# Three edits to the first batch of a fused attention, token-mixer and channel-mixer kernel

## The reference, cut to what matters

```python
for t in range(S):                                  # attention, per batch and head
    state = alpha[:, :, t, :, None] * state + np.einsum('bhd,bhe->bhde', k[:, :, t], v[:, :, t])
    y[:, :, t] = np.einsum('bhd,bhde->bhe', q[:, :, t], state)

xt = x.transpose(0, 2, 1)                           # token mixer, then channel MLP
h = np.maximum(xt @ w_tok1, 0.0) @ w_tok2
u = x + h.transpose(0, 2, 1)
x = u + np.maximum(u @ w_ch1, 0.0) @ w_ch2

xk = mu_k * x + (1.0 - mu_k) * x_prev               # channel mix, x_prev is x one token earlier
xr = mu_r * x + (1.0 - mu_r) * x_prev
k = np.maximum(xk @ w_k, 0.0)
out = 1.0 / (1.0 + np.exp(-(xr @ w_r))) * (k * k @ w_v)
```

## Time and profile before

| | before |
|---|---|
| median of 3 runs | 732.86 us (732.38 to 733.08) |
| the profiled execution | 732.64 us |
| its span in the trace | 730.9 us |
| PE busy | 725.4 us (99%) |
| DVE busy | 472.2 us (65%) |
| ACT busy | 331.1 us (45%) |
| POOL busy | 197.2 us (27%) |

### The profile page before, as it was taken

How to read it: one execution, slowest core, us unless ns; L and a number is a source line. 1 busy time by engine, 2 the same in 40 slices (tenths; PEclk the granted TensorE clock), 3 DMA queues, 4 the chain that set the end, 5 groups by cost and what they waited for, 6 DMA issues and landing times.

```text
span 730.9 us, 13853 instructions
## 1 busy us (share of the span) xinstructions
PE 725.4 (99%) x4556; PEld 719.3 (98%) x4556; DVE 472.2 (65%) x1298; ACT 331.1 (45%) x953; POOL 197.2 (27%) x344
## 2 busy tenths in 40 slices
PE   9999999999999999999999999999999999999998
PEld 8999999999999999999999999999999999999998
DVE  7988888865888875888883412446457365473561
ACT  5866544432544442444442332436346264373550
POOL 3875564333243331334432440310000000000000
PEclk9999999999999999999999999999999999999999
DMA  9973535542425544243531224010011010110000
GB/s 205 220 153 77 97 56 108 85 72 65 56 42 86 103 82 77 49 55 56 111 62 33 87 86 141 33 33 34 33 54 44 33 38 28 52 43 32 11 22 32
DMA packets 210187, 50.90 MB, mean 70 GB/s; under 512 B 190416, under 2 KB 207312, under 8 KB 210128
## 3 DMA queue, kind: packets, MB, share of 16 engines
q1 hardware_dynamic: 206992, 45.05, 30.9%
q0 software_dynamic: 1152, 4.72, 1.8%
q10 hardware_dynamic: 1984, 0.41, 0.3%
HBM read 37.17 MB, written 12.98 MB: 69 GB/s over the span
## 4 chain that ended last, share of the span: by engine, by line
PE 96%; SPq 1%; DMA 1%; DVE 1%; ACT 0%; issue 0%; DVEq 0%
PE bank L798 21%; PE bank L814 21%; PE bank L894 14%; PE bank L872 14%; PE bank L881 5%; PE bank L716 5%; PE bank L684 4%; PE bank L786 3%; PE bank L755 3%; PE bank L721 2%; PE bank L714 2%; PE bank L679 1%; SPq L351 1%; PE bank L767 1%; PE bank L692 1%; PE bank L656 1%
## 5 line engine op out<-in xcount | busy, mean ns | idle before, releaser
L991 ACT ACTIVATE hid_hi<-bank 128x384 fp32r<-128x384 f32 x96 | 47.2, 492 | 115.5 <-PE bank L798 115.2
L1257 DVE SCALAR_TENSOR_TENSOR hid_lo<-bank,hid_hi 128x384 fp32r<-128x384 f32 x96 | 53.2, 555 | 65.5 <-ACT hid_hi L991 64.5
L1091 ACT ACTIVATE relu_k<-bank 128x384 f32<-128x384 f32 x64 | 31.5, 492 | 106.0 <-PE bank L872 86.1
L798 PE MATMUL bank<-u_hi,wch_hi 128*128 128x384 f32 x288 | 72.1, 358 | 0.0
L798 PE MATMUL bank<-u_lo,wch_hi 128*128 128x384 f32 x288 | 66.3, 338 | 0.0
L814 PE MATMUL bank<-hid_lo,wch_hi 128*128 128x384 f32 x288 | 65.5, 334 | 0.0
L798 PE MATMUL bank<-u_hi,wch_lo 128*128 128x384 f32 x288 | 65.4, 334 | 0.0
L814 PE MATMUL bank<-hid_hi,wch_hi 128*128 128x384 f32 x288 | 65.4, 334 | 0.0
L814 PE MATMUL bank<-hid_hi,wch_lo 128*128 128x384 f32 x288 | 65.4, 334 | 0.0
L1391 DVE TENSOR_TENSOR x_half<-bank,x_half 128x384 f32<-128x384 f32 (+2 forms) x25 | 13.5, 541 | 77.4 <-PE bank L894 75.3
L567 POOL TENSOR_SCALAR_AFFINE_SELECT relu_k<-relu_k 128x256 f32<-128x256 f32 x72 | 29.3, 407 | 112.2 <-ACT relu_k L973 112.2
(11 more groups left out here) (141 smaller groups left out, 1833.3 us busy)
## 6 DMA issues: line engine op xcount, KB each, us to landing
w_raw<-in_moe_w_ch SPq DMA_DIRECT2D x12, 384.0 KB, 3.6
x_scratch<-x_half POOLq DMA_DIRECT2D x8, 576.0 KB, 3.6
out<-x_half SPq DMA_DIRECT2D x23, 192.0 KB, 1.9
vt<-in_v SPq DMA_DIRECT2D x48, 72.0 KB, 2.3
x_scratch<-x_sum SPq DMA_DIRECT2D x18, 192.0 KB, 2.1
x_sum<-x_scratch SPq DMA_DIRECT2D x72, 48.0 KB, 2.2
qka<-in_q SPq DMA_DIRECT2D x49, 48.0 KB, 2.2
qka<-in_alpha SPq DMA_DIRECT2D x49, 48.0 KB, 2.2
```

The costliest lines, as they stand in the source:

```text
L798: mm = nc.tensor.matmul(dst, ch1_w(a, n % KC, jj), u[c][:, n % KC, half * HT:(half + 1) * HT], start=(n == 0), stop=(n == 3 * KC - 1))
L991: nc.scalar.activation(dst, b_ring[t % 2][:, 0:HT], func).then_inc(tile_hi, 1)
L1257: ins = nc.vector.scalar_tensor_tensor(dst, src, 0.0, hi, ALU.max, ALU.subtract)
```

## The change

1. **Start.** Alpha of the first pair is the first load on SP, k the second; q of the first pair is the first on ACT's queue. PE turns alpha first, into a bank of its own, and signals it (`first_alpha_done`); the two scans of step 0 wait for this alone. Two fill passes stand between alpha's transpose and those of q and k. The fill is made of transposes in place of products, with new counts.
2. **Weights.** The 20 half pieces are spread over the slots 4 to 25 (none in 11 and 19), and POOL's whole pieces stand in slots 5, 7, 9, 12, 14, 16, 18, 21, 23 and 25. SP loads piece 1 ahead of chunk 2. The loads of mu and DVE's use of them move behind the head and the batches.
3. **x^T of the first token half of batch 0** goes through DRAM: SP stores three groups of rows in slot 16 and loads the blocks of one group in each of slots 20, 21 and 22 (four transfers each); DVE turns them in slots 25 to 27 and adds them in `down_base`. The nine PE transposes of this half are gone. The second half stays as it was. The loads of batch 1's first half block are spread over slots 16 to 19, and those of the second stand behind the loop and mu.

```diff
+        def transposed_alpha(r, i):
+            return bank[2][0:W2, 0:P] if is_first(r) and i == 0 else transposed_qka(r, i)[:, 2 * P:3 * P]
...
+        def half_slot(j):
+            return FIRST_UNIT + (STEPS - 1) * j // (2 * CH1_END)
         def pieces_in(s):
-            bounds = [min(max(n - 3, 0) * CH1_END // (STEPS - NP), CH1_END) for n in (s, s + 1)]
-            return range(*bounds)
+            return [n for n in range(CH1_END) if half_slot(2 * n + 1) == s]
...
+            def store_first_x():
+                sp.wait_ge(xlo_ready, NP * TM)
+                for m in range(KC):
+                    sp.dma_start(x_rows[0][m].rearrange("(c p) f -> p c f", p=P),
+                                 x_sum[:, 0:TM, m * P:(m + 1) * P]).then_inc(first_rows_stored, 16)
+            def load_first_x_blocks(m):
+                sp.wait_ge(first_rows_stored, 16 * KC)
+                for a in range(4):
+                    sp.dma_start(x_sum[32 * a:32 * (a + 1), m, :].rearrange("p (n j) -> p n j", j=32),
+                                 x_rows[0][m].rearrange("(n p) (a j) -> a p n j", p=32, j=32)[a])\
+                      .then_inc(first_raw_loaded[m], 16)
...
-            for n, t in ((0, q), (2, alpha)):
+            for n, t, loaded in ((2, alpha, alpha_pair_loaded), (1, k, pair_loaded)):
...
-            for c in range(1, 3):
-                load_qka(c)
-                load_piece(c - 1)
-                load_v(c)
+            load_qka(1)
+            load_piece(0)
+            load_v(1)
+            load_piece(1)
+            load_qka(2)
+            load_v(2)
             load_piece(2)
-            for n, m in enumerate((mu_k, mu_r)):
...
-                if s % NP == 0 and s >= NP * (NC - 2) and s < STEPS:
-                    load_half(1, s // NP - NC + 2)
-                if s % NP == 3 and s >= NP * (NC - 2) and s < STEPS:
-                    load_half_v(1, s // NP - NC + 2)
+                n = s - NP * (NC - 2)
+                if n == 0:
+                    store_first_x()
+                if 0 <= n < 3:
+                    load_half(1, 0, (n,))
+                elif n == 3:
+                    load_half_v(1, 0)
+                elif 4 <= n < 4 + KC:
+                    load_first_x_blocks(n - 4)
                 for n in pieces_in(s):
                     load_piece(n + NRAW)
+            for n, m in enumerate((mu_k, mu_r)):
+                sp.dma_start(mu[:, n, :], m.rearrange("(c p) -> p c", p=P),
+                             allow_slow_non_contiguous=True).then_inc(mu_loaded, 16)
+            load_half(1, 1)
+            load_half_v(1, 1)
...
-            WARM = (4, 4, 2, 3, 2, 1, 1)
+            WARM = (8, 5, 2, 6, 4, 2, 2)
...
-                for n in range(3):
+                for n in (2, 0, 1):
+                    if i == 0 and n == 0:
+                        pe.wait_ge(pair_loaded, 32)
...
+                    if i == 0 and n == 2:
+                        mm.then_inc(first_alpha_done, 1)
+                        keep_warm(2)
...
-                if b == 0:
+                turned_by_pe = b == 0 and half == 1
+                if turned_by_pe:
...
-                    nc.tensor.matmul(b_ring[1][:, 0:P], ident[:, :], ident[:, :], start=True, stop=True)
+                    nc.tensor.transpose(b_ring[1][:, 0:P], ident[:, :], ident[:, :])
...
-                n, half = divmod(s - 3, 2)
-                if 0 <= n < CH1_END:
-                    split_half_hi(n, half)
+                for j in range(2 * CH1_END):
+                    if half_slot(j) == s:
+                        split_half_hi(*divmod(j, 2))
...
+            def turn_first_x(m):
+                dve.wait_ge(first_raw_loaded[m], 64)
+                nc.vector.transpose(x2_half[0][:, m, :], x_sum[:, m, :]).then_inc(first_turned, 1)
...
-                if b == 0:
+                if b == 0 and half == 0:
+                    dve.wait_ge(first_turned, m + 1)
+                    ins = nc.vector.tensor_tensor(x2_half[0][:, m, :], src, x2_half[0][:, m, :], ALU.add)
+                elif b == 0:
                     ins = nc.vector.tensor_copy(x2_half[half][:, m, :], src)
...
+                if STEPS + 1 <= s <= STEPS + KC:
+                    turn_first_x(s - STEPS - 1)
```

More of the change, by code:

```diff
@@ L177, in attention_mixer_channel_mix @@
         omu_ready = sem("omu_ready")
+        alpha_pair_loaded = sem("alpha_pair_loaded")
         pair_loaded = sem("pair_loaded")
@@ L184, in attention_mixer_channel_mix @@
         w_lo_ready = sem("w_lo_ready")
+        first_alpha_done = sem("first_alpha_done")
         tr_done = sem("tr_done")
@@ L214, in attention_mixer_channel_mix @@
         x_turned = sem("x_turned")
+        first_rows_stored = sem("first_rows_stored")
+        first_raw_loaded = [sem(f"first_raw_loaded{n}") for n in range(KC)]
+        first_turned = sem("first_turned")
         x2_stored = [sem(f"x2_stored{n}") for n in range(2)]
@@ L359, in load_v, with load_half @@
                              v[0, :, c * P:(c + 1) * P, :].rearrange("h p d -> p h d")).then_inc(v_loaded[buf], 16)
-            def load_half(r, n):
+            def load_half(r, n, tensors=range(3)):
                 buf = buffers(r, TM * n)[0]
@@ L370, in load_half @@
                     sp.wait_ge(turned, TM * (before - 1))
-                for a, t in enumerate((q, k, alpha)):
+                for a in tensors:
                     for lane, h, d0, d1, f0 in GROUPS:
                         sp.dma_start(blocks[buf][lane:lane + 32, a, :, f0:f0 + d1 - d0],
-                                     t[r, 2 * p + h, ts, d0:d1].rearrange("(t p) d -> p t d", p=32))\
+                                     (q, k, alpha)[a][r, 2 * p + h, ts, d0:d1].rearrange("(t p) d -> p t d", p=32))\
                           .then_inc(qka_loaded[buf], 16)
@@ L410, in load_piece @@
                 sp.dma_start(dst.rearrange("p (k n) -> p k n", k=piece_size(n)[0]), PIECES[n][0]).then_inc(loaded, 16)
-            for n, t in ((0, q), (2, alpha)):
+            for n, t, loaded in ((2, alpha, alpha_pair_loaded), (1, k, pair_loaded)):
                 sp.dma_start(qka3[0][n][:, 0:2, 0:D], t[0, 0:2, 0:P, :].rearrange("h p d -> p h d"))\
-                  .then_inc(pair_loaded, 16)
+                  .then_inc(loaded, 16)
             sp.dma_start(qka3[0][0][:, 2:H, 0:D], q[0, 2:H, 0:P, :].rearrange("h p d -> p h d"))\
@@ L649, in transposes @@
                     pe.wait_ge(consts_v, 2)
-                    pe.wait_ge(pair_loaded, 48)
+                    pe.wait_ge(alpha_pair_loaded, 16)
                 if i % NP == (1 if i < NP else 0):
@@ L654, in transposes @@
                     pe.wait_ge(qkd_ready, i - 1)
-                for n in range(3):
-                    mm = nc.tensor.transpose(
-                        transposed_qka(r, i)[:, n * P:(n + 1) * P], qka3[qb][n][:, 2 * p:2 * p + 2, :].rearrange("p h d -> p (h d)"), ident[:, :])
+                for n in (2, 0, 1):
+                    if i == 0 and n == 0:
+                        pe.wait_ge(pair_loaded, 32)
+                    dst = transposed_alpha(r, i) if n == 2 else transposed_qka(r, i)[:, n * P:(n + 1) * P]
+                    mm = nc.tensor.transpose(dst, qka3[qb][n][:, 2 * p:2 * p + 2, :].rearrange("p h d -> p (h d)"),
+                                             ident[:, :])
+                    if i == 0 and n == 2:
+                        mm.then_inc(first_alpha_done, 1)
+                        keep_warm(2)
                 mm.then_inc(tr_done, 1)
@@ L786, in token_down @@
                     mm = nc.tensor.matmul(dst, h1[i][:, kt, m * P:(m + 1) * P], tok2_w(j, kt, half),
-                                          start=(b > 0 and n == 0), stop=(n == 3 * KT - 1))
+                                          start=(n == 0 and not turned_by_pe), stop=(n == 3 * KT - 1))
                 mm.then_inc(tile_done, 1)
@@ L1047, in mix_next @@
                         mix_step(nxt, half, n, 0, KC - 1)
-            act.dma_start(qka3[0][1][:, 0:2, 0:D], k[0, 0:2, 0:P, :].rearrange("h p d -> p h d"))\
+            act.dma_start(qka3[0][0][:, 0:2, 0:D], q[0, 0:2, 0:P, :].rearrange("h p d -> p h d"))\
                .then_inc(pair_loaded, 16)
-            for n, t in ((1, k), (2, alpha)):
+            for n, t in ((2, alpha), (1, k)):
                 act.dma_start(qka3[0][n][:, 2:H, 0:D], t[0, 2:H, 0:P, :].rearrange("h p d -> p h d"))\
@@ L1140, in scans @@
             def scans(r, i):
-                alphaT = transposed_qka(r, i)[:, 2 * P:3 * P]
+                alphaT = transposed_alpha(r, i)
                 if i >= 4:
                     dve.wait_ge(state_sum, NST * r + updates(r, i - 3))
-                if is_first(r):
+                if is_first(r) and i == 0:
+                    dve.wait_ge(first_alpha_done, 1)
+                elif is_first(r):
                     dve.wait_ge(tr_done, i + 1)
@@ L1156, in scale_qk @@
                 G = STEPS * r + i
+                if is_first(r) and i == 0:
```

(7 more changed lines are left out.)

2 lines of the change are left out of this document (removed).

## The result

The changed kernel takes 736.53 us (735.70 to 737.83, 6 executions) against 732.97 us for the kernel before (732.38 to 733.91): ratio 1.0049, 95% interval 1.0039 to 1.0059. It is slower by 0.5%, 3.6 us. The forecast was 732.4 with a range up to 734.8, so the time lies outside it. The profiled execution took 737.53 us, with a span of 735.8; it is one of the three with the lowest mean granted clock (0.995, 736.78 to 737.83 us), and the other three, at 0.997 and 0.998, took 735.70 to 736.28. So the trace shows more of the loss (4.9 us against the profiled execution of before) than the median has.

What follows compares the result with a forecast made beforehand. DVE was taken to bound the head until about 51 us, PE from there on. The terms -0.14 - 0.32 + 0.95 - 0.99 = -0.50 us took 732.86 to 732.4 us, range 731.0 to 734.8.

Steps and rivals of the forecast that it cites:

- the paragraph on x^T: End of the head: three transpose triples leave PE, -0.99 us; DVE's turns fit its 2.08 us wait, loads in time, cost 0.
- x^T lands late: Rival, end of the head: third group lands at 56, PE waits about 1 us more, +0.5, 733.4 us; chance 0.09.
- the clock rises late: Rival, slots 2 to about 6: transposes delay the fast clock, 733.6 to 735.6 us; chance 0.21, or 0.03 slow throughout head.
- The start: Step 0's scans start earlier, step 1 still waits for all of chunk 0; shorter PE fill before the first mask: -0.14 us.
- The weights: Spread of weight halves in the head: -0.32 us for DVE's stall, +0.95 for POOL's late low part.
- The stall near 17 us: DVE's state update at 17.39 starts at 17.07, as ACT's half of piece 1 moves a slot later: -0.32 us.
- POOL's last low part: End of the head: step 23's low part, behind later weight pieces, ends at 54.8 in place of 53.84: +0.95 us.
- The transposes: Three triples of x^T transposes leave PE's stream in `token_down`: -0.99 us, bounded from below by 0.6.
- the sum of -0.50: Whole kernel: start -0.14, stall -0.32, POOL +0.95 and transposes -0.99 us added together, chance 0.53.

Runs made afterwards that it cites:

- e3_fill_gap: The changed kernel with 24 more fill transposes on PE between the first token product and the next scores: 734.70 us, ratio 1.0026 to the kernel before.
- e5_late_products: e2_turn_late with the fill made of products in place of transposes, about as many passes: 732.66 us, ratio 0.9998 to the kernel before.
- e7_start_only: The kernel before with the first edit (start) alone: 732.84 us, ratio 0.9996 to the kernel before.
- e10_xt_only: The kernel before with the third edit (x^T through DRAM) alone: 736.30 us, ratio 1.0033 to the kernel before.
- e2_turn_late: The changed kernel with DVE's third turn moved behind the low parts of q and h and slot 1's work: 732.48 us, ratio 0.9995 to the kernel before.
- e1_no_xt: The changed kernel with its third edit undone, x^T of the first half from PE's transposes again: 733.37 us, ratio 1.0008 to the kernel before.
- e4_old_spread: The changed kernel with the weight halves back in slots 3 to 22: 734.45 us, ratio 1.0029 to the kernel before.
- e9_quiet_landing: The changed kernel with the two 384 KB weight loads behind the third group's blocks waiting for the turns: 736.34 us, ratio 1.0036 to the kernel before.

## Why the prediction was wrong

**The step that failed** is the paragraph on x^T: "They must not wait for their data", with its estimate that the third group's loads "are issued around 49 to 51 us and land 2.2 later", at 53, and "nothing is lost". They were issued from 52.38 to 54.38 and landed at 57.5. Of the 4.5 us, some 3.4 are SP's line: I counted it from 35 us with every transfer at the 0.5 us of the cheapest group of four. The block loads did take 0.5 each, but the line began at 35.67 (0.7), the first half block's q took 2.94 and its k 2.41 in place of 2.0 each (1.3), its two loads of v 1.81 in place of 1.0 (0.8), and the stores and the small gaps between all of them make up the rest (0.6). A queue that was never idle had no slack to take this up, with 15 more transfers in its line. The other 1.0 is the landing: 3.2 us in place of 2.2, between weight loads. The cost was set at 0 and is +3.1 until PE goes on, plus 2.25 for the clock behind it in the profiled execution; by the medians the two are 2.3 and 1.7.

**The rival was there, but too small and too unlikely.** "x^T lands late" named the mechanism, the place and the wait of DVE, with +1 of PE's wait and 733.4 us, at a chance of 0.09. It landed 1.5 us later than even this case assumed. And it had no second term: that PE, after standing still for 3 us, came back at half its clock, which cost 1.7 us more by the medians and 2.25 in the profiled execution. Both missing parts are of the same sign, and together they carry the time over the range.

**The clock.** The rival "the clock rises late" gave the range its upper end, and it is refuted. In the changed kernel all passes on PE before 7.0 us are transposes, of fill or of data, and the rise is not late. The 3 transposes at 6.43 take 0.54 us, less than the 0.63 of two at 4.12, so PE is fast at 6.4 us, where the kernel before was still slow (four fill passes in 0.98 us from 6.52) and was fast only from about 7.6:

```profile
4.12 0.63 PE L693 MATMUL bank<-ident,qka 128*96 128x128 f32 x2
...
6.43 0.54 PE L693 MATMUL bank<-ident,qka 128*96 128x128 f32 x3 [0.61 <-DMA qka<-in_k]
...
7.10 0.62 PE L719 MATMUL bank<-x_half,qkd 96*128 96x256 f32 x2
```

The Trainium skill (TensorE: Matmul & The Clock Gate, section PE-mode transpose) says that the full clock doesn't engage for transposes. For the float32 transposes of this kernel the trace disagrees, as does e3_fill_gap, where transposes alone held the granted clock at 1.00; e5_late_products, with products as fill, is fast at 6.21 and takes the same time. The measurement decides.

**The start.** -0.14 was right: the scan of step 0 came 0.6 us earlier (4.01 in place of 4.60), and that of step 1 at 7.00, as before 6.98, since it waits for the last tensor of chunk 0. The first mask came at 8.29, 1.29 after it as forecast, and 0.12 earlier than before. By time alone e7_start_only can't show so small a term.

**The weights.** The stall near 17 us went, -0.34 for a forecast of -0.32 (from one scan to the next 15.74 to 17.52, in the trace of before 15.78 to 17.90). But DVE lost some 0.3 us at 39.95, in a wait that the profile puts down to no engine. It isn't the weights' doing, since e7_start_only and e10_xt_only have it too (at 40.04 and 40.65); its cause is open. POOL's last low part ended at 54.54 in place of 53.84, so +0.70 for a forecast of +0.95 less 0.46 gained before, +0.49; the 0.3 lost at 39.95 are about the difference. The wait stood where it was forecast.

**The transposes.** -0.99 was right: e2_turn_late against e1_no_xt, which differ by them and the way round through DRAM, is 0.9995 against 1.0008, -0.95 us, and every execution of the one (at most 732.84) is faster than every one of the other (at least 732.95) on the same chip.

Without the failed step the sum of -0.50 was good: e2_turn_late, which is the change without it, measures -0.0005 of 733, -0.4 us (-1.0 to +0.3). Some of that closeness is luck: the unexplained 0.3 us stand in it, and chunk 0 landed 0.24 us earlier in its profiled execution than in that of before.

## What to carry to other kernels

When a producer is moved off the critical engine, ask where its consumer stands in the order of the helper engine: an instruction that waits for a transfer belongs behind everything that PE needs sooner, however short it is. Count a queue's issue time before adding transfers to it; here, one that issued without pause for 20 us delayed each new transfer by all those in front of it. And price a wait of several microseconds on PE twice, once for the wait (2.3 us here) and once for the slower clock after it (1.7). Look at the granted clock of each execution and not only at the median: in e4_old_spread and e10_xt_only it sorted the times.

## What the runs showed of the hardware

- With a wait of 2.97 us on PE (55.9 to 58.9 us) the granted clock fell to 0.50 (1.2 GHz) at about 57.0 and stayed there until about 63.8, though PE was busy from 58.9 on. A wait of 2.4 us (e4_old_spread) left it at 1.00 in the profiled execution, but six of that kernel's twelve executions had a mean clock below 1.00. With one of 2.7 us (e10_xt_only) it was 0.50 for some 3.4 us, from about 58.5. From the scores to the first channel unit PE took 9.68 us at the full clock (e3_fill_gap), 11.16 with the 3.4 us (e10_xt_only) and 11.93 with the 6.8 us (the changed kernel).
- Transposes of an identity held the clock at 1.00 (e3_fill_gap) and raised it at the start as products did: PE was fast at 6.43 us with a fill of transposes and at 6.21 with one of products (e5_late_products), and the ratios were 0.9995 and 0.9998.
- With two 384 KB loads issued right behind four of 48 KB these had landed 3.2 us after the last issue (the changed kernel), with none behind 2.3 (e9_quiet_landing), both with a 384 KB load just in front; with none just in front and one behind it was 1.6 (e4_old_spread). SP issued the block loads of 48 KB in 0.47 us each, one every 0.51.
